# Attention pooling and soft mixture chain: the query pair sums prepared one head earlier, the maximum jobs at other score steps, and the half query tile transposed at full rows

## The reference, cut to what is computed

```python
q_pool = q.reshape(B, H, S // 2, 2, D).mean(axis=3)      # S = 1152, D = 64
scores = scale * np.matmul(q_pool, k.transpose(0, 1, 3, 2))
scores = scores - np.max(scores, axis=-1, keepdims=True)
attn = np.exp(scores)
attn = attn / (np.sum(attn, axis=-1, keepdims=True) + 1e-09)
out = np.matmul(attn, v)
```

## Time and profile before

| what | value |
|---|---|
| median of 3 runs | 786.74 us (784.47 to 787.75) |
| the profiled execution's own time | 786.78 us |
| its span (first to last instruction) | 785.0 us |
| PE busy | 752.6 us of the span (96%) |
| POOL, DVE, ACT busy | 488.5, 481.0, 394.9 us |
| mean granted TensorE clock | 0.992 of full speed |

### The profile page before, as it was taken

The page is one execution under the profiler, slowest core; times in us unless marked ns, Lnnn a source line. Parts: engine busy times, 40 slices in busy tenths (PEclk is TensorE's granted clock), DMA queues, the critical chain, the costliest instruction groups (busy, mean ns, idle before and its releaser), DMA issues.

```text
span 785.0 us, 16851 instructions
## 1 busy us (share of the span) xinstructions
PE 752.6 (96%) x6397; PEld 546.6 (70%) x6397; DVE 481.0 (61%) x773; ACT 394.9 (50%) x784; POOL 488.5 (62%) x399
## 2 busy tenths in 40 slices
PE   4999999999999999999999989898899999999996
PEld 2777776777767767777677766432488888888885
DVE  6677676776766767767677637521575455555541
ACT  1465564664655646556465553211565454545452
POOL 1578888788887888878888772100475444444442
PEclk9999999999999999999999999999899999999999
DMA  3223324334243242333433208399700110101011
GB/s 82 81 70 85 108 84 148 99 99 149 82 139 109 89 148 93 120 127 83 149 98 102 87 22 305 147 364 387 267 1 10 32 28 14 40 0 40 1 40 41
DMA packets 51622, 81.82 MB, mean 104 GB/s; under 512 B 14557, under 2 KB 20573, under 8 KB 51549
## 3 DMA queue, kind: packets, MB, share of 16 engines
q1 hardware_dynamic: 51548, 80.83, 32.9%
HBM read 75.94 MB, written 4.79 MB: 103 GB/s over the span
## 4 chain that ended last, share of the span: by engine, by line
PE 91%; DVE 3%; DMA 2%; POOL 1%; issue 1%; ACT 1%; SPq 0%; ACTq 0%; POOLq 0%
PE ps L567 18%; PE ps L778 8%; PE ps L779 8%; PE ps L777 8%; PE ps L547 8%; PE ps L517 6%; PE ps L549 5%; PE ps L551 5%; PE ps L553 5%; PE ps L578 2%; PE ps L482 2%; PE ps L767 2%; PE ps L696 2%; PE ps L487 2%; DMA w_in<-in_moe_w_in 2%; PE ps L720 1%
## 5 line engine op out<-in xcount | busy, mean ns | idle before, releaser
L426 POOL TENSOR_TENSOR p_sum<-p_sum,probs 128x576 f32<-128x576 f32 x160 | 251.2, 1570 | 23.2 <-POOL p_sum L426 0.4
L1070 DVE TENSOR_REDUCE mx<-ps 128x2 f32<-128x1024 f32 (+1 forms) x160 | 191.3, 1221 | 102.0 <-PE ps L517 101.8
L848 ACT ACTIVATE probs<-ps 128x576 f32<-128x576 f32 x288 | 183.7, 652 | 43.2 <-PE ps L553 42.2
L455 POOL TENSOR_TENSOR g_lo<-g_buf,g_hi 128x384 fp32r<-128x384 f32 x96 | 100.5, 1048 | 103.5 <-ACT g_hi L978 103.4
L567 PE MATMUL ps<-probs,v_sb 128*64 128x288 f32 x1152 | 146.8, 409 | 0.7 <-ACT probs L848 0.7
L567 PEld LDWEIGHTS ps<-probs,v_sb 128*64 128x64 f32 x1152 | 79.9, 137 | 55.3 <-ACT probs L848 1.0
L1267 DVE SCALAR_TENSOR_TENSOR v_buf<-u_buf 128x384 f32<-128x384 f32 x96 | 58.8, 613 | 91.3 <-ACT u_buf L971 91.1
L779 PE MATMUL ps<-wo_lo,g_hi 128*128 128x512 f32 x288 | 113.6, 394 | 0.0
L778 PE MATMUL ps<-wo_hi,g_lo 128*128 128x512 f32 x288 | 113.4, 394 | 0.0
L777 PE MATMUL ps<-wo_hi,g_hi 128*128 128x512 f32 x288 | 113.0, 392 | 0.0
L547 PE MATMUL ps<-q_hi,k_hi 64*128 64x288 f32 x576 | 107.7, 359 | 0.9 <-ACT probs L848 0.9
(11 more groups left out here) (182 smaller groups left out, 1085.5 us busy)
## 6 DMA issues: line engine op xcount, KB each, us to landing
pre<-in_moe_w SPq DMA_DIRECT2D x47, 512.0 KB, 5.3
k_raw<-in_k SPq DMA_DIRECT2D x32, 288.0 KB, 4.0
v_sb<-in_v SPq DMA_DIRECT2D x32, 288.0 KB, 2.9
q_raw<-in_q SPq DMA_DIRECT2D x32, 256.0 KB, 3.8
from_x<-in_moe_w SPq DMA_DIRECT2D x9, 512.0 KB, 4.5
out<-o_stage SPq DMA_DIRECT2D x36, 128.0 KB, 2.4
p_inv<-inv_dram SPq DMA_DIRECT2D x62, 72.0 KB, 2.6
staged<-in_moe_w SPq DMA_DIRECT2D x8, 512.0 KB, 6.1
```

The costliest lines, as they stand in the source:

```text
L426: nc.gpsimd.tensor_tensor(total, total, probs[:, u, :], ALU.add).then_inc(probs_added, 1)
L848: nc.scalar.activation(dst, ps[:, b0:b0 + 2, 0:HALF], ACT.Exp, scale=SCORE_SCALE).then_inc(exp_done, 1)
L1070: top = nc.vector.tensor_reduce(mx[0:w, NC * t:NC * t + 2], ps[0:w, b:b + 2, :], AX.X, ALU.max)
```

## The change

The pair sums and their copy are made one head earlier and at another place in each engine's program. POOL runs prepare(n + 3) after the six additions of head n, where it ran prepare(n + 2) before them. ACT runs double_q(n + 3) between the rounding copies and read_x(n), where it ran double_q(n + 2) after the exponential of step 4. SP loads the queries of head n + 3 in loop n instead of those of head n + 2, after the keys of head n + 2. At the start the sums and the copy of head 2 are made as well. The maximum jobs move from steps 0, 1, 3, 5, 6, 8 to steps 0, 2, 3, 4, 6, 7. The half query tile is transposed with all 128 rows (the lower 64 hold zeros).

```diff
-            def load_k_q(m):
+            def load_k(m):
                 if m > 0:
                     sp.wait_ge(turned, 2 * m)
                 sp.dma_start(k_raw[:, 0:NT, :], k_dram[m]).then_inc(k_loaded, 16)
                 sp.dma_start(k_raw[:, NT, :], k_dram[m][:, NT - 1, :]).then_inc(k_loaded, 16)
+
+            def load_q(m):
                 if m > 0:
                     sp.wait_ge(q_pooled, m)
...
-            load_k_q(0)
-            load_k_q(1)
+            load_k(0)
+            load_q(0)
+            load_k(1)
+            load_q(1)
...
             for n in range(HEADS):
+                if n == 0:
+                    load_q(2)
                 if n + 2 < HEADS:
-                    load_k_q(n + 2)
+                    load_k(n + 2)
+                if n + 3 < HEADS:
+                    load_q(n + 3)
...
                 if n > 1:
+                    pool.wait_ge(q_pooled, min(n + 3, HEADS))
                     divide_x(n - 2)
-                if n + 2 < HEADS:
-                    prepare(n + 2)
...
+                if n + 3 < HEADS:
+                    prepare(n + 3)
...
             prepare(1)
+            prepare(2)
...
-            JOB_STEPS = (0, 1, 3, 5, 6, 8)
+            JOB_STEPS = (0, 2, 3, 4, 6, 7)
...
-                    mm = pe.transpose(ps[:, tail_bank(m), P:P + QLAST], 
-                                      q_pool[0:QLAST, QF, :, :].rearrange("p two d -> p (two d)"), ident[0:QLAST, 0:QLAST])
+                    mm = pe.transpose(ps[:, tail_bank(m), P:2 * P],
+                                      q_pool[:, QF, :, :].rearrange("p two d -> p (two d)"), ident[:])
...
             round_k_q(1)
+            double_q(2)
             for n in range(HEADS):
                 for s in range(NT):
                     exp_step(n, s)
-                    if s == 4 and n + 2 < HEADS:
-                        double_q(n + 2)
                 if n + 2 < HEADS:
                     round_k_q(n + 2)
+                if n + 3 < HEADS:
+                    double_q(n + 3)
                 if n + 1 < HEADS:
                     read_x(n)
```

## The result

The changed kernel takes 774.1 us (median of 4 runs, 771.94 to 774.61) against 786.8 us: ratio 0.984, 95% interval 0.981 to 0.987. It is faster, but by 12.7 us where 6.7 were forecast, and outside the range. The profiled execution's span is 772.6 us against 785.0.

What follows compares the result with a forecast made beforehand. PE's own chain, 14.11 us per head, was taken as the bound, with POOL just inside. Less 0.19 and 0.03 gives 13.89; in total 5.7 + 0.9 + 0.1 = 6.7 us off 786.78, so 780 us, range 777 to 783.

Steps and rivals of the forecast that it cites:

- The delay of exponential 0: On ACT, the copy now ahead of x_raw makes exponential 0 start 0.16 us later per head, bounds 0.05 to 0.35.
- What bounds: PE's own chain sets the head at 14.11 us; POOL ends 0.13 us before add_up and never holds PE there.
- Removed changes of shape: PE's transposes: full rows remove two tile-shape changes, 0.19 us per head in 30 heads, 5.7 us; bounds nothing to 0.19.
- Moved pair sum and copy: POOL loses nothing; on ACT the copy before read_x waits for prepare, making exponential 0 0.16 us late.
- Moved maximum jobs: PE's score steps: new job places pay back the 0.16 us delay and 0.03 more, 0.9 us over 29 heads.
- POOL and the pair addition: POOL's last addition is delayed by DVE's pair addition, so POOL's end follows DVE's start and stays 0.13 us before add_up.
- 0.60 plus the offset: POOL's additions end late by about 0.60 us plus the offset between DVE's pair-addition start and the POOL addition's start.
- The later spread of the sums: On SP, the spread starts near 2.3 instead of 1.55 us after add_up; if late, 0.40 us plus job 5's lead covers.
- The rivals: Gain partly eaten, 785 us (0.22); copy's chain becomes the bound, 793 us (0.10); POOL becomes the bound, 790 us (0.08).
- The third: POOL becomes the bound: add_up at 14.24 us, 29 x 0.10 = 2.9 us plus slower spread, about 790 us; chance 0.08.

Runs made afterwards that it cites:

- The cut addition: The kernel before with POOL's sixth addition cut from 576 to 8 columns; 784.9 us, ratio 0.999.
- the kernel with the later sum: The changed kernel with POOL's pair sum of a head put behind divide_x instead of ahead of it; 829.9 us, ratio 1.056.
- The cut pair addition: The kernel before with DVE's pair addition cut from 576 to 8 columns; 786.3 us, ratio 1.000.
- the second trace: The whole change run once more, nothing altered, beside the kernel without the moved sums on one chip; 774.8 us, ratio 0.985.

## Why the prediction was partly right, and where it failed

The mechanism was mostly right; two terms of the sum had the wrong size. The delay of exponential 0 was put at 0.16 us per head and was 0.01, so that the moved maximum jobs gained 0.16 instead of 0.03. The removed changes of shape were put at 0.19 and were 0.24. Together this is the difference between the 0.22 forecast and the 0.40 measured per head.

**What bounds.** Right: PE's own chain, with POOL 0.13 us inside it. The cut addition showed it, and weigh to add_up is 4.52 in all heads up to 29 but the three in which POOL stands still. What the sum left out is that POOL becomes the bound in head 30 (4.94) and counts in head 31.

**Removed changes of shape.** The mechanism was right, the term too small: 0.19 forecast, 0.24 measured (8.0 us for the part alone, against 5.7). The 0.19 between the transposes was met exactly; the 0.05 between the transpose of the maxima and weigh was not in the sum; the earlier trace rows show 0.25 there, and it is 0.20 behind a full transpose.

**Moved pair sum and copy.** This step failed in its size. "exponential 0 about 0.30 after x_sum's start, 1.85, against 1.69: late by 0.16" was measured as 1.70. The error is in the hand-overs. The pair sum starts 0.18 before add_up, where 0.06 before it was taken, and lasts 0.86 instead of 0.88; the copy, x_raw and x_sum follow at 0.38 and 0.29 instead of 0.39 and 0.31; and behind x_sum the chain needs 0.26 instead of 0.30, by the kernel with the later sum. So the chain would allow exponential 0 at 1.64, and step 0's scores hold it to 1.70, as before. The stated bounds (0.05 to 0.35) did not reach down to zero. That the same place holds a chain which can set the head was right: moved alone the sums cost 7 us, and made 1.78 us later they cost about 55 us, of which some 13 belong to the lower clock.

**Moved maximum jobs.** "So the delay of 0.16 is paid back and 0.03 more" fell with it. Without any delay, the same working gives a gain of 0.17 (0.03, and the 0.14 by which step 2 was taken to be late); measured are 0.16 between the two heads laid beside each other, and 0.20 for the jobs alone (14.14 to 13.94, means). The reason given was right: step 1 follows step 0 at once, and step 3 no longer waits for exponential 1. What was wrong is to which part the gain belonged: I treated the moves as one trade, in which the jobs pay for the sums. Run apart, the jobs gain 6.8 us and the sums lose 7.0 us, and together the loss all but vanishes, since it was job 1's wait ahead of step 1.

**POOL and the pair addition.** Right: the delay of the last addition follows the offset of DVE's start. In the changed kernel DVE starts at 130.82, 0.28 before the addition's nominal start (124.86 + 6.24 = 131.10). By "0.60 plus the offset" the five would end 0.32 late; they end 0.31 late (7.97 - 7.66). The cut pair addition showed the cause. This is also why a faster PE was not stopped by POOL in the ordinary heads. In head 30, where DVE starts 0.76 after the third of the five (444.90 against 444.14), its own addition takes 1.26 instead of 0.74.

**SP.** The later spread of the sums did no harm. In four heads v's issue took 1.80 to 2.40 us, and in three of them DVE waited 0.16 to 0.36 us for the spread sums that stand behind it; two of those heads are no longer than the others, and the third, head 17, is as long in the second trace, where DVE has no such wait. So there was cover.

**The rest.** From the add_up of head 0 to that of head 29 the whole change saves 11.7 us (435.43 - 36.96 = 398.5 against 448.08 - 37.94 = 410.1), 0.40 per head. The first add_up came 1.0 us sooner (36.96 against 37.94), head 30 gives 0.2 and head 31 takes 0.5 back: 12.4 us, the difference of the two spans. The 1.0 at the start is in part chance, since the same kernel run again has its first add_up at 37.62; there the whole change was worth 11.0 us (774.8 against 785.8). The rivals: none came true. The third, POOL as the bound, shows in the three odd heads, in head 30 and in head 31. Its price had a slip: 14.24 against 14.11 is 0.13 per head and 3.8 us, not 0.10 and 2.9.

**Open.** Why the gap behind the score steps stays when a transpose of the same tile shape follows; why ACT's x_raw starts 0.29 us late in head 16 of the kernel before; and why POOL stands still for 0.28 us in heads 10, 17 and 24 and before its sixth addition in head 31. From one of POOL's places to the next there are 64 of POOL's shown instructions (nine in most heads).

## What to carry to other kernels

When a change moves several things, price each alone at its old surroundings too: here one part alone was a loss of 7 us that another part, moved for its own gain, made almost free. The two parts without it do as well as all three (773.3 against 774.8 us on one chip). For a new chain of hand-overs, let the lower bound be zero delay where the engine it feeds was itself waiting. When an engine is made to wait, look at the granted clock too before the whole loss is put down to the wait. A wait that the view puts down to another engine counts only if the same interval gets shorter when that engine is early; compare it in a head where the engine is plainly early, and look whether the bracket stands on PE or only on PEld.

## What the runs showed of the hardware that was not expected

- One more 64-row transpose costs 0.36 us among full ones, where it changes the tile shape twice, and 0.07 us beside its like. The Trainium skill (TensorEngine Tiling, Key Properties) says that changing the tiling mode drains TensorE; these two prices agree with it. The effect reaches over the next transpose: 0.33 instead of 0.27 us, and 0.05 more before the matmul behind.
- POOL's pair sum, which doesn't depend on the addition ahead of it, starts before that one's shown end (119.08 against 119.12), while additions that depend on each other stand 0.14 us apart (1.56 from start to start at 1.42 each). The Trainium skill (Perfetto Trace Analysis, GPSIMD Engine Instruction) advises to time GpSimd by the spacing of starts rather than by the shown spans; these rows bear it out.
- DVE's and POOL's additions exclude each other. How much POOL loses hangs on the offset: 0.31, 0.40 and 0.79 us for starts of DVE 0.28 and 0.17 before and 0.20 after POOL's. The Trainium skill (SBUF — State Buffer, SBUF: two separate sides) says that whichever starts first has the shared ports for its whole instruction and the other blocks. The exclusion agrees; the order does not at the last offset, by the shown starts: POOL's starts 0.20 us earlier and loses 0.79, while DVE's takes its usual 0.75. With 8 columns, at the same offset, DVE is the one that waits (1.22 us).
